# First-chunk routing logits: column-group products with a turned sum in place of twelve small products

## The reference, cut to what matters

```python
def _moe2_ref(x, w_gate, w1, w2, capacity):
    logits = x @ w_gate                      # 1152 x 512 times 512 x 8
    expert_idx = np.argmax(logits, axis=1)
    probs = softmax(logits)                  # written out in the original
    gate_w = probs[np.arange(N), expert_idx]
    # each token takes the next free place of its expert, up to capacity;
    # h = relu(disp @ w1), y = h @ w2, out[i] = gate_w[i] * y[expert, place]
```

## Time and profile before

| | us |
|---|---|
| median of three runs | 313.29 (313.15 to 313.43) |
| profiled execution, its own time | 313.66 |
| its span | 311.8 |
| PE busy | 301.3 (97%) |
| DVE busy | 219.7 (70%) |
| ACT busy | 153.2 (49%) |
| POOL busy | 138.0 (44%) |

### The profile page before, as it was taken

The page is one execution under the profiler, slowest core; times in us unless marked ns, Lnnn a source line. Parts: engine busy times, 40 slices in busy tenths (PEclk is TensorE's granted clock), DMA queues, the critical chain, the costliest instruction groups (busy, mean ns, idle before and its releaser), DMA issues.

```text
span 311.8 us, 7143 instructions
## 1 busy us (share of the span) xinstructions
PE 301.3 (97%) x2761; PEld 251.0 (80%) x2761; DVE 219.7 (70%) x583; ACT 153.2 (49%) x337; POOL 138.0 (44%) x155
## 2 busy tenths in 40 slices
PE   7899999999999999999999999999999999999793
PEld 6566676676677988878999989898989889987572
DVE  5899998999978366997784547857765498862300
ACT  1777866767866144655641543545344564203020
POOL 4777997998998300555780012015031332300121
PEclk9999999999999999999999999999999999999999
DMA  8998889761547600000001309650043048029980
GB/s 152 164 211 201 220 154 193 192 173 43 159 115 175 204 0 2 0 2 2 0 2 18 59 4 366 203 83 3 2 68 48 0 163 376 4 104 360 383 319 11
DMA packets 75049, 38.50 MB, mean 123 GB/s; under 512 B 66009, under 2 KB 66017, under 8 KB 73989
## 3 DMA queue, kind: packets, MB, share of 16 engines
q1 hardware_dynamic: 72340, 36.74, 44.5%
q10 hardware_dynamic: 2416, 0.59, 1.1%
q0 software_dynamic: 256, 0.67, 0.6%
HBM read 32.66 MB, written 5.39 MB: 122 GB/s over the span
## 4 chain that ended last, share of the span: by engine, by line
PE 91%; DVE 2%; issue 2%; SPq 2%; DMA 1%; ACT 0%; POOL 0%; POOLq 0%; DVEq 0%
PE bank_a L1851 17%; PE bank_b L1851 16%; PE bank_out L1808 6%; PE bank_b L1911 4%; PE bank_pt L1761 4%; PE bank_pt L1911 4%; PE bank_a L1709 4%; PE bank_a L1785 3%; PE bank_a L2083 2%; PE bank_out L1884 2%; PE bank_b L2083 2%; PE bank_out L1805 2%; PE bank_b L1704 2%; PE bank_out L2216 2%; PE bank_b L2093 2%
## 5 line engine op out<-in xcount | busy, mean ns | idle before, releaser
L717 POOL TENSOR_SCALAR prob<-prob,rl,gate_loc 128x512 f32<-128x512 f32 (+3 forms) x64 | 41.7, 666 | 11.9 <-DVE rl L1243 11.9
L1851 PE MATMUL bank_a<-x_hi,win_hi 128*128 128x288 f32 x128 | 39.3, 307 | 0.0
L1851 PE MATMUL bank_b<-x_hi,win_hi 128*128 128x288 f32 x128 | 38.1, 297 | 0.0
L1851 PE MATMUL bank_b<-x_lo,win_hi 128*128 128x288 f32 x128 | 38.0, 297 | 0.0
L1851 PE MATMUL bank_a<-x_hi,win_lo 128*128 128x288 f32 x128 | 38.0, 297 | 0.0
L1851 PE MATMUL bank_b<-x_hi,win_lo 128*128 128x288 f32 x128 | 38.0, 297 | 0.0
L1851 PE MATMUL bank_a<-x_lo,win_hi 128*128 128x288 f32 x128 | 37.9, 296 | 0.0
L972 ACT ACTIVATE g_raw<-bank_a,biases 128x576 f32<-128x576 f32 x16 | 11.9, 743 | 50.6 <-DVE sq L1320 50.6
L909 ACT ACTIVATE prob<-prob,negmax 128x512 f32<-128x512 f32 (+3 forms) x64 | 35.0, 550 | 0.8 <-DVE negmax L1193 0.8
L809 POOL TENSOR_TENSOR w_lo<-w_sb,w_hi 128x512 fp32r<-128x512 f32 x8 | 11.4, 1426 | 48.0 <-ACT w_hi L1015 48.0
L1326 DVE TENSOR_TENSOR g_raw<-g_raw,sq 128x576 f32<-128x576 f32 x32 | 31.6, 987 | 0.5 <-ACT sq L973 0.5
(11 more groups left out here) (332 smaller groups left out, 800.0 us busy)
## 6 DMA issues: line engine op xcount, KB each, us to landing
w_sb<-in_moe_w_dram SPq DMA_DIRECT2D x6, 2048.0 KB, 11.4
win_raw<-in_moe_w_in_dram SPq DMA_DIRECT2D x4, 1024.0 KB, 5.6
wout<-in_moe_w_out_dram SPq DMA_DIRECT2D x4, 1024.0 KB, 5.9
win_raw<-in_moe_w_in_dram SPq DMA_DIRECT2D x1, 4096.0 KB, 13.7
out_dram<-zero_row SPq DMA_DIRECT2D x8, 288.0 KB
x_d<-x_rows SPq DMA_DIRECT2D x32, 72.0 KB, 2.1
v_sb<-in_v_dram SPq DMA_DIRECT2D x16, 128.0 KB, 2.5
qn<-in_q_dram SPq DMA_DIRECT2D x24, 72.0 KB, 5.5
```

Source lines behind the costliest of these rows:

```text
L717: pool.tensor_scalar(prob[u][:, h, :], prob[u][:, h, :], rl[:, c:c + 1], gate_loc[:, 2 * j + h:2 * j + h + 1], ALU.mult, ALU.mult).then_in ...
L1851: last = pe.matmul(h_bank(d)[:, t, :], w[:, m, f:f + P], x[c % 2][:, m, :], start=(m == 0 and n == 0), stop=(m == KT - 1 and n == 2))
```

## The change

`first_logits` now runs after block 2 of chunk 1 instead of after block 3. It makes four products in column groups, one for each quarter of the model width. The gate, padded with zeros from 8 to 32 columns (`wg_pad`), holds the array as weights, and `x2T` with 288 tokens moves through it. The result lies in `bank_t`, transposed, as four partial sums. DVE copies it to `lgT`, behind the clip of block 3. PE's `token_logits(1)`, after block 3, sums the four groups with `sel`. `wg_pad` is made by POOL, behind `few_iota`, in the bytes of the zero rows. `logits(1, 0)` waits for the copy of `lgT` instead of for `wp`.

```diff
@@ gpsimd, behind few_iota
+            pool.memset(wg_pad[:, :, :], 0.0).then_inc(s_pad, 1)
+            pool.wait_ge(s_pad, 1)
+            pool.wait_ge(s_wg, 16 * 5)
+            pool.tensor_copy(wg_pad[:, :, 0:E], wg[:, :, :]).then_inc(s_pad, 1)
             x_lo_part(2)
@@ vector, chunk(c, first)
+                    if c == 1 and d == 3:
+                        dve.wait_ge(s_xl1, 1)
+                        dve.tensor_copy(lgT[:, :], bank_t[:, 0:CHUNK]).then_inc(s_xle, 1)
                     if c > 1 and d == 2:
                         copy_lt(c)
@@ tensor, logits(c, q)
                 if q == 0:
-                    pe.wait_ge(s_wpe, 1)
+                    pe.wait_ge(s_xle, 1)
@@ tensor, first_logits()
                 pe.wait_ge(s_ye, KT)
-                for r in range(NR):
-                    for m in range(KT):
-                        last = pe.matmul(bank_o[0:ST, LG_AT + r * E:LG_AT + (r + 1) * E], x2T[:, m, r * ST:(r + 1) * ST], wg[:, m, :],
-                                         start=(m == 0), stop=(m == KT - 1))
-                last.then_inc(s_lg, 1)
+                pe.wait_ge(s_pad, 2)
+                pe.wait_ge(s_wpe, 1)
+                for m in range(KT):
+                    last = pe.matmul(bank_t[32 * m:32 * m + 32, 0:CHUNK], wg_pad[:, m, :], x2T[:, m, :], start=True, stop=True)
+                last.then_inc(s_xl1, 1)
@@ tensor, token_logits(c)
-                pe.wait_ge(s_lte, c - 1)
+                if c == 1:
+                    pe.wait_ge(s_xle, 1)
+                else:
+                    pe.wait_ge(s_lte, c - 1)
@@ tensor, chunk(c, first)
-                    if c == 1 and d == 3:
+                    if c == 1 and d == 2:
                         first_logits()
-                    if c > 1 and d == 3:
+                    if c > 0 and d == 3:
                         token_logits(c)
```

More of the change, by code:

```diff
@@ L189, in build_program @@
         hot = [sb(f"hot{n}", [ST, NR, P], BF16, at=(wg_rep_at, zero_at)[n // 2] + 2 * NR * P * (n % 2))[0] for n in range(NCH)]
+        wg_pad, _, _ = sb("wg_pad", [P, KT, 32], F32, at=zero_at)
         few_iota, _, _ = sb("few_iota", [ST, P], F32, at=zero_at + 4 * NR * P)
@@ L379, in build_program @@
         s_fio = sem("s_fio")
+        s_pad = sem("s_pad")
+        s_xl1 = sem("s_xl1")
+        s_xle = sem("s_xle")
         s_list = sem("s_list")
```

## The result

| | before | changed |
|---|---|---|
| median, 15 runs each on the same chips | 312.87 us (312.30 to 313.68) | 313.49 us (312.99 to 314.12) |
| profiled execution, its own time | 313.66 | 314.01 |
| its span | 311.8 | 312.1 |
| PE busy | 301.3 (x2761) | 301.1 (x2751) |

The changed kernel takes 1.002 times the time of before (95% interval 1.0012 to 1.0028), which is 0.4 to 0.9 us more, around 0.62. Beside the experiments it was measured once more, with the ratio 1.0022 (1.0013 to 1.0032). So it is a little slower, at the bound that I had set for what can be told. One of the twelve executions of the experiment "weights early, on before" took 1358 us and counts as slow; its ratio leaves that one out.

A forecast was written before the change was run, and what follows sets the result against it. PE was taken as the bound, with 91% of the span and no waits around the change. Terms: -2.06 + 0.82 + 0.53 + 1.34 = +0.63, tail -0.29, net +0.34 on 313.29: 313.6 us, range 312.7 to 314.2.

The forecast's parts named there:

- The old products: Between blocks 3 and 4, PE's twelve routing-logit products in 24 rows go, saving 2.06 us.
- the first new block: Behind block 2, four products in column groups, 8 rows side by side, cost PE 0.82 us.
- the wait: Between blocks 3 and 4, PE stands without cover for DVE's clip and copy: 1.34 us, bounds 1.2 and 1.8.
- the work alone: On PE in chunk 1, products removed and added, without any standing: -2.06 + 0.82 + 0.53 = -0.71 us.
- the turned sum costs 0.53: Behind block 3, three products summing the groups, 6 rows, cost PE 0.53 us, read from the next chunk.
- the tail: At the kernel's end, PE's instruction stops fall 9 product rows later in the work, giving back 0.29 us.
- the second stop: PE's 0.82 us stop before the last 57 rows of L2216 would stand before the last 48, ending 0.29 us earlier.
- rival 2: In the tail, the 1.59 us stop moves under cover, gaining about 1.0 us: 312.9, or 312.6 with 0.29 more; 18%.
- the first stop: PE's 1.59 us stop before the last 2 rows of L2182, read as running out of instructions at a fixed place.
- the likeliest case: Whole kernel: no measurable change with a slight loss, 313.6 us, own range 313.3 to 313.9; 45%.
- Rival 1: PE's standing after block 3 costs its full price, the kernel's end gives nothing back: 313.9, at most 314.4; 27%.
- Rivals 3 and 4: After block 3 no standing shows, 312.6, 7%; behind block 2 the column groups don't run side by side, 315.8, 3%.

The follow-up runs named there:

- weights early, on before: Kernel before, with the first further expert's second weights asked for before SP waits for the few hidden products; ratio to before 1.0002.
- copy early: Changed kernel with DVE's copy of the logits behind block 2's clip instead of block 3's; ratio to before 0.9953, second time 0.9970 on another chip.
- sum after block 4: Changed kernel with PE's turned sum moved from behind block 3 to behind block 4, DVE's copy left in place; ratio to before 0.9970.
- copy early, with the wait: Changed kernel with DVE's copy behind block 2's clip, PE's turned sum still waiting for block 3's clip; ratio to before 1.0005.
- both edits together: Changed kernel with DVE's copy behind block 2's clip and the further expert's second weights asked for earlier; 311.24 us, ratio to before 0.9947.

## Why the prediction was right, and where it was not

**Right: which way the sum goes, and what carries it.** The old products went for 2.06 us, the first new block cost 0.81 (forecast 0.82), and the wait stood where I put it, because PE's next instruction hangs on DVE's copy behind a clip that PE itself releases. Taking the wait away turned the loss into a local gain of 0.66, and of 0.72 counted from the end of block 2, against the 0.71 that I had worked out for the work alone. POOL and the earlier place cost nothing that can be measured, as worked out.

**Mis-sized: the wait.** I took 1.34 us; it is 1.50. From row to row it is 1.51, which is 1.38 more than a step: 0.04 more than the terms of the earlier trace rows give, of which 0.03 are the copy (0.45 for 0.42). Another 0.08 is that the sum's own rows take longer after a stand: from their first row to the second of block 4 are 0.75 us in the changed kernel, against 0.67 with the copy early. The last 0.04 is spread over blocks 4 and 5, and no row names it. With it the local loss is 0.84 instead of 0.63. The step "the turned sum costs 0.53" was read from a place where PE did not come from a stand.

**Near in size by luck, wrong in its working: the tail.** I had the tail give back 0.29 us through the second stop, and set rival 2, the first stop moving under cover, aside. In fact the first stop did move and that stretch (from the product by `wout` to `few_first`) fell from 7.30 to 5.79 us, more than the 1.0 of rival 2. The second stop, nine rows later in the work, on which the 0.29 rests, is in no trace. The reason I gave against rival 2 was the right one in kind: what PE won it lost again in waiting, only the wait is for the weights' landing and not for instructions. Between local loss and measured loss lie 0.15 to 0.22 us for the changed kernel. Three of the other kernels with its instruction count and the weights unmoved agree (0.28, 0.28 and 0.30: copy early the second time, sum after block 4, copy early with the wait); the first copy early gives 0.81 and does not. In four of these five the local difference lies inside the measured interval, and in the fifth 0.02 us outside it, so it is their common sign that speaks. I take the tail to give back 0.2 to 0.3 us, as an estimate.

**The forecast** of 313.6 (+0.34) against a measured +0.62 is the result of a wait too small by 0.16, the 0.06 in blocks 1 and 2 that no term foresaw, and a tail that gives back a little less than I said. The measured +0.62 lies at the edge of the likeliest case's own range, and so near only because a tail that works otherwise than I had it gives back nearly what I had written for it. Rival 1, the wait at full price and nothing back from the tail, predicted 313.9 or +0.63. In the number it was as near as could be, but it took the wait at 1.34 and nothing back from the tail; with a local loss of 0.84 and 0.2 back, two errors cancel in it. Rivals 3 and 4 fell with the first trace.

**Open.** A trace is one execution, and the kernel before has only one, in which the second stop shows. Its tail takes 28.25 us; the two kernels with the old count and no added wait, where it doesn't show, take 27.30 and 27.35 (the second with the weights early), and the changed kernel 27.60 and 27.41. So against the one the tail gives back 0.65 to 0.84 us and against the others it takes 0.1 to 0.3 more. To give back 0.2 to 0.3 on average, the stop would have to come in about half of the executions of before; that is an estimate from these traces, and no run counts it. Copy early won 1.47 us on one chip and 0.94 on another, but its own medians are 312.30 and 312.13; it is the kernel before that took 313.56 and 313.00. Why is open.

## What to carry to other kernels

Before a product is split into a product, a copy and a second product, ask where in the copying engine's list the copy stands: behind an instruction that waits for the engine which will wait for the copy, it costs that engine the whole chain, and one place earlier, or one block of work in between, it costs nothing. Then ask what the end of the program hangs on after the change, since a load issued from inside the tail can take back what the matrix engine wins there; both edits together gave 1.7 us where neither the changed kernel nor the weights alone gave any.

## What the runs showed of the hardware that I had not expected

In the trace with a stand of 1.24 us followed by 2.0 us of products of 8 columns the granted clock fell to half in the next block, which cost 1.5 us on top of the stand, and by the mean clock it fell in seven of nine executions; after a stand of 1.51 us followed by 0.5 us of them it fell in none of 26. A stop of PE lies at a fixed count of its rows (2451 or 2452) in all fourteen traces, whatever the program does there, and takes 0.28 to 1.79 us of idle; PE goes on 2.2 to 2.5 us after an instruction packet starts. Nine idle transposes less at the start cost 2.4 us until block 1, and the first entry of a full clock comes at 14.8 us instead of 6.6, which the views don't show.
